# LSH attention and mixture of experts on one core: rows kept in two float16 parts, expert operands turned by the DMA crossbar, five-step weight turns

## The reference

```python
q_bits = (np.einsum('bhsd,dk->bhsk', q, proj) > 0)      # k alike; 6 bits give a bucket
mask = q_bucket[:, :, :, None] == k_bucket[:, :, None, :]
scores = np.where(mask, scale * q @ k.T, -1e9)
attn = softmax(scores);  x = attn @ v                    # rows of all heads: (2, 768, 512)

logits = x @ w_gate                                      # 8 experts
local_gate = sigmoid(x @ w_local)
for s in range(S):                                       # for each batch entry
    e = argmax(logits[s]) if s == 0 or local_gate[s] < 0.5 else prev_e
    h = np.maximum(x[s] @ w1[e], 0.0)                    # 512 -> 1024
    out[s] = softmax(logits[s])[e] * (h @ w2[e])         # 1024 -> 512
```

## Time and profile before

| what | value |
|---|---|
| median of 3 runs | 520.87 us (520.6 to 522.49) |
| the profiled execution | 521.36 us, its span 519.6 us |
| mean granted TensorE clock | 0.971 |
| busy: TensorE, VectorE, ScalarE, GpSimd | 94%, 56%, 57%, 64% of the span |
| chain that ended last | PE 62%, POOL 12%, ACT 10%, DVE 5%, issue 5%, DMA 2% |

### The profile page before, as it was taken

One profiled execution on the slowest core, in us unless ns is written; L12 is line 12 of the kernel. 1 busy time (PEld: TensorE's weight loads), 2 busy tenths in 40 slices (PEclk: granted clock), 3 DMA queues, 4 the chain that ended last, 5 costly groups with the idle time before them and its releaser, 6 DMA issues.

```text
span 519.6 us, 11257 instructions
## 1 busy us (share of the span) xinstructions
PE 486.6 (94%) x4396; PEld 296.3 (57%) x4396; DVE 289.0 (56%) x421; ACT 294.8 (57%) x275; POOL 329.9 (64%) x179
## 2 busy tenths in 40 slices
PE   6889999799999999998878799999999999999994
PEld 2457767477676766676753455555555555555551
DVE  5776566456566666653758554455445554455451
ACT  3278878667868787887874330768585675000000
POOL 1248868849796978879361893499696969500001
PEclk9999999799999999999957999999999999999998
DMA  7665766236563623200092325646638280200000
GB/s 196 149 167 142 215 161 161 74 90 161 161 162 94 183 58 78 50 4 2 9 358 91 100 80 171 257 171 237 232 122 314 60 330 22 112 13 20 7 1 0
DMA packets 54979, 65.11 MB, mean 125 GB/s; under 512 B 30531, under 2 KB 39119, under 8 KB 54930
## 3 DMA queue, kind: packets, MB, share of 16 engines
q1 hardware_dynamic: 45438, 44.22, 28.4%
q10 hardware_dynamic: 6452, 12.05, 7.7%
q0 software_dynamic: 3040, 8.13, 5.0%
HBM read 47.99 MB, written 8.13 MB: 108 GB/s over the span
## 4 chain that ended last, share of the span: by engine, by line
PE 62%; POOL 12%; ACT 10%; DVE 5%; issue 5%; DMA 2%; SPq 1%; ACTq 0%; DVEq 0%; POOLq 0%
PE pA L1254 18%; PE pO L1254 18%; POOL room L505 7%; ACT room L710 5%; POOL W L374 4%; PE pB L1287 3%; ACT room L716 3%; PE pA L578 2%; PE pA L577 2%; PE pB L595 2%; PE pB L594 2%; DMA room<-in_k 1%; PE pP L1244 1%; ACT W L366 1%; PE pO L637 1%
## 5 line engine op out<-in xcount | busy, mean ns | idle before, releaser
L505 POOL TENSOR_TENSOR room<-room 128x1536 f16<-128x1536 f32 x46 | 142.6, 3103 | 56.9 <-ACT room L716 56.7
L374 POOL TENSOR_TENSOR W<-room,W 128x1024 f16<-128x1024 f32 x64 | 135.4, 2135 | 30.9 <-ACT W L366 29.6
L804 DVE TENSOR_REDUCE room<-pA 128x2 f32<-128x1536 f32 x46 | 80.8, 1757 | 51.5 <-PE pA L578 51.3
L360 ACT ACTIVATE room<-W 128x1024 f32<-128x1024 f32 x64 | 64.8, 1048 | 75.1 <-DMA W<-in_moe_w 43.4
L1254 PE MATMUL pA<-W,room 128*128 x432 | 96.2, 379 | 0.4 <-DVE room L1341 0.4
L1254 PE MATMUL pO<-W,room 128*128 x432 | 96.3, 379 | 0.0
L710 ACT ACTIVATE room<-pB 128x1536 f32<-128x1536 f32 x48 | 69.4, 1445 | 43.4 <-PE pB L595 41.4
L716 ACT ACTIVATE room<-room 128x1536 f16<-128x1536 f32 x48 | 71.2, 1484 | 1.5
L1254 PEld LDWEIGHTS pA<-W,room 128*128 128x128 f16 x432 | 42.3, 98 | 47.5 <-issue 0.7
L1254 PEld LDWEIGHTS pO<-W,room 128*128 128x128 f16 x432 | 42.3, 98 | 46.9
L366 ACT ACTIVATE W<-room 128x1024 f16<-128x1024 f32 x64 | 64.9, 1049 | 0.8
(11 more groups left out here) (206 smaller groups left out, 664.7 us busy)
## 6 DMA issues: line engine op xcount, KB each, us to landing
W<-in_moe_w SPq DMA_DIRECT2D x24, 1024.0 KB, 9.6
room<-room SPq DMA_DIRECT2D x93, 96.0 KB, 2.2
W<-in_moe_w ACTq DMA_DIRECT2D x8, 1024.0 KB, 5.8
room<-in_q SPq DMA_DIRECT2D x16, 192.0 KB, 3.4
W<-in_v ACTq DMA_DIRECT2D x4, 768.0 KB, 5.7
x_rows<-XN SPq DMA_DIRECT2D x12, 256.0 KB, 3.4
room<-in_k SPq DMA_DIRECT2D x15, 192.0 KB, 3.9
room<-room SPq DMA_DIRECT2D x31, 18.0 KB
```

The costliest lines, as they stand in the source:

```text
L374: pool.tensor_tensor(parts(r)[:, 1, cols], FULL[:, place(r), cols], parts(r)[:, 0, cols], ALU.subtract).then_inc(s_ready, 1)
L505: pool.tensor_tensor(PTL[:, n % NP, :, :], E32[:, n % 2, :, :], PTH[:, n % NP, :, :], ALU.subtract).then_inc(s_lo, 1)
L804: dve.reduce_max(RM[:, g % 2, 2 * p:2 * p + 2], scores_in(n)[:, :].rearrange("p (i s) -> p i s", i=2), AX.X).then_inc(s_rmax, 1)
```

## The change

1. `norm` writes XN as two float16 parts, already scaled: the result stays in PSUM, then a high copy and a low difference go to XNS. That is five dependent instructions where there were three.
2. `turn_rows` turns both parts (eight float16 transposes into one PSUM block seen as float16), and one copy per row block (`copy_rows`) replaces the high and low instructions; of row blocks 4 to 11 the even ones are copied by ScalarE, the odd ones by VectorE.
3. x_rows holds the float16 parts, so gathered tiles need no split.
4. In the expert stage x and h are turned by DMA transposes that SyncE issues (`turn_x`, one per tile for both parts of x; `turn_h`, one for each part of h; each moves 128 x 1,024 float16, 256 KB). VectorE makes both parts of h before the turn (`split_h`: high part, relu in place in PSUM, low part). TensorE's order becomes up(t+1), down(t). Only the first x and the last h are still turned by TensorE.
5. In attention a weight quarter is split in turns of five steps that begin at step 9; `scale_weights` waits for one half of the low parts at a time; loads go out one head later; the last V split moves from head 3 to head 2. r = 7 is split mostly after the router.
6. The loads of experts 3 to 7 are issued by ScalarE between its splits, two at most in advance, after the down product of the expert's last tile.

```diff
-        V_HEADS, V_SUMS = (-1, 0, 1, 3), (0, 2, 3, 5)
+        V_HEADS, V_SUMS = (-1, 0, 1, 2), (0, 2, 3, 5)
...
+        W_STEPS, W_AT = 5, 9
...
         def turn_rows(pe, i):
...
-            for d in range(DC):
-                last = pe.transpose(pG[buf][:, d * P:(d + 1) * P], XN[:, c, d * P:(d + 1) * P], idf[:, :])
+            for a in range(2):
+                for d in range(DC):
+                    last = pe.transpose(pG[buf][:, a, d * P:(d + 1) * P], XNS[:, c, a, d * P:(d + 1) * P], idh[:, :])
...
+        def copy_rows(eng, i):
             _, buf, before = logits_of(i)
+            eng.wait_ge(s_gt, i + 1)
+            wait(eng, s_gl, before)
+            if by_act(i):
+                eng.activation(XTC[:, buf, :, :], pG[buf], ACT.Copy).then_inc(s_gha, 1)
             else:
+                eng.tensor_copy(XTC[:, buf, :, :], pG[buf]).then_inc(s_gc, 1)
...
-            wait(act, s_ready, 2 * (r if r <= EARLY else r - 1))
+            wait(act, s_ready, 2 * (r if r <= EARLY else r - 1) - 1 + half)
...
-                if h > 2 and h % 2 == 1 and p > 0 and h // 2 <= EARLY:
-                    low_weights(pool, h // 2 - 1, p - 1)
+                r, u = (n - W_AT) // W_STEPS, (n - W_AT) % W_STEPS
+                if 0 <= r < EARLY and u >= 3:
+                    low_weights(pool, r, u - 3)
...
-                if p == 2 and h < V_PARTS:
-                    if h == V_RAW:
+                if p == 2 and 0 <= h - 1 < V_PARTS:
+                    if h - 1 == V_RAW:
                         act.wait_ge(s_vl, NG)
-                    load_weights(act, h)
-                r, u = (h - 2) // 2, (h - 2) % 2 * PAIRS + p
+                    load_weights(act, h - 1)
+                r, u = (n - W_AT) // W_STEPS, (n - W_AT) % W_STEPS
...
-                dst = XN[:, :, :].rearrange("p (j b) n -> p j (b n)", j=J)[:, :, g * D:(g + 1) * D]
-                dve.tensor_tensor(dst, po[:, :, 0:D], REC[:, :].unsqueeze(2).to_broadcast([P, J, D]),
-                                  ALU.mult).then_inc(s_x, 1)
+                chain.link(dve.tensor_tensor(po[:, :, 0:D], po[:, :, 0:D], REC[:, :].unsqueeze(2).to_broadcast([P, J, D]),
+                                             ALU.mult))
+                hi, lo = (XNS.rearrange("p (j b) a n -> p j b a n", j=J)[:, :, g // H, a, g % H * D:(g % H + 1) * D]
+                          for a in range(2))
+                chain.link(dve.tensor_copy(hi, po[:, :, 0:D]))
+                dve.tensor_tensor(lo, po[:, :, 0:D], hi, ALU.subtract).then_inc(s_x, 1)
...
+            def turn_x(t):
+                sp.wait_ge(s_xin[t], 16)
+                wait(sp, s_h, t - 1)
+                sp.dma_start_transpose(XT[:, t % 2, :, :].rearrange("p a (d n) -> p (a d) n", n=P),
+                                       XIN16[:, t, :]).then_inc(s_xt[t % 2], 16)
+
+            def turn_h(t):
+                for a, s in ((0, s_hhi), (1, s_hlo)):
+                    sp.wait_ge(s, t + 1)
+                    wait(sp, s_y, t - 1)
+                    sp.dma_start_transpose(HT[:, t % 2, a, :].rearrange("p (f n) -> p f n", n=P),
+                                           HN[:, a, :]).then_inc(s_ht[a][t % 2], 16)
+
+            turn_x(1)
+            for t in range(NT - 1):
+                turn_h(t)
+                if t + 2 < NT:
+                    turn_x(t + 2)
...
+                pe.wait_ge(s_xt[t % 2], turned(t) - (16 if t % 2 == 0 else 0))
+                wait(pe, s_hlo, t)
...
+                    for a in range(2):
+                        pe.wait_ge(s_ht[a][t % 2], turned(t))
...
-            for t in range(1, NT - 2):
+            for t in range(NT - 2):
                 up(t + 1)
-                xt(t + 2)
                 down(t)
-                ht(t + 1)
...
+                act.wait_ge(s_y, ends[e])
+                r0 = 4 * (e + RING)
+                load_weights(act, r0)
+                for r in range(r0, r0 + 4):
+                    if r + 1 < r0 + 4:
+                        load_weights(act, r + 1)
+                    split_weights(r)
...
+            def split_h(t):
+
                 dve.wait_ge(s_h, t + 1)
...
+                dve.tensor_scalar(HN[:, 0, :], pH[:, 0:F], 0.0, HSC / (XS * WS), ALU.max, ALU.mult).then_inc(s_hhi, 1)
+                dve.tensor_scalar(pH[:, 0:F], pH[:, 0:F], 0.0, HSC / (XS * WS), ALU.max, ALU.mult).then_inc(s_hr, 1)
+                dve.wait_ge(s_hr, t + 1)
...
+                dve.tensor_tensor(HN[:, 1, :], pH[:, 0:F], HN[:, 0, :], ALU.subtract).then_inc(s_hlo, 1)
```

More of the change, by code:

```diff
@@ L276, in logits_of, with by_act, copied @@
             return (i - half) * B + 1, i % 3, i - 1 if i < half + 2 else 0 if i == half + 2 else i - 2
+        def by_act(i):
+            return i >= NS - TAIL and i % 2 == 0
+        def copied(eng, i):
+            if by_act(i):
+                eng.wait_ge(s_gha, sum(by_act(k) for k in range(i + 1)))
+            else:
+                eng.wait_ge(s_gc, sum(not by_act(k) for k in range(i + 1)))
         def turn_rows(pe, i):
             c, buf, before = logits_of(i)
-            wait(pe, s_gc, before)
-            for d in range(DC):
-                last = pe.transpose(pG[buf][:, d * P:(d + 1) * P], XN[:, c, d * P:(d + 1) * P], idf[:, :])
+            if before > 0:
+                copied(pe, before - 1)
+            for a in range(2):
+                for d in range(DC):
+                    last = pe.transpose(pG[buf][:, a, d * P:(d + 1) * P], XNS[:, c, a, d * P:(d + 1) * P], idh[:, :])
             last.then_inc(s_gt, 1)
@@ L1327, in _, with split_weights @@
         def _(act):
-            for r in range(EARLY + 2, NR):
+            def split_weights(r):
                 scale_weights(act, r, 0)
```

206 lines of the change are left out of this document (90 added, 116 removed).

## The result

| | change | before, same session |
|---|---|---|
| median (20 runs each) | 521.91 us | 521.48 us |
| lowest to highest | 510.58 to 540.89 | 519.49 to 526.95 |
| profiled execution, its span | 530.44, 528.4 us | 521.36, 519.6 us |
| mean granted clock | 0.957 | 0.971 |

The forecast was 504.3 us, range 490 to 514. The medians are equal. The ratio is 0.9861 [0.9811, 0.991]; it is taken over each kernel's lowest runs alone, within 1.5% of its lowest, and for the change these are four of the twenty. So the change won some 1.4% when it went well, and nothing in its middle run; instead the runs, 7.5 us apart before, are 30 us apart now. The profiled execution is one of the long ones, 8.5 us above the median. It shows well what goes wrong, but its waits are larger than those of the middle run.

A forecast was written before the change was run, and what follows sets the result against it. TensorE was taken to bound the expert stage and, nearly, attention. The terms -22.1 + 0.9 + 3.4 - 7.5 + 9.3 - 1.1 = -17.1 took 521.36 to 504.3 us, range 490 to 514.

The forecast's parts named there:

- term 1: Expert stage: x and h turns leave TensorE, the cycle falls from 11.67 to 10.37 us; -22.1 us.
- It fits: Expert stage: three DMA turns of 3.4 us each on SP's queue keep up with a 10.37 us cycle.
- rival C: Expert stage: SP's queue does one turn at a time and becomes the bound; 557.5 us at 4.5 us each; chance 0.12.
- rival B: Expert stage: weights come late because turns and loads share DMA engines; +8.6, 512.9 us; chance 0.10.
- Term 2: Entry to the expert cycle: second up product waits for three VectorE instructions, +0.9 us, then a clock fall, +3.4 us.
- The fall of the clock: Entry to the expert cycle: TensorE idles about 3.1 us, then runs at half clock; +3.4 us, bounds 0 and 3.4.
- Term 3: Attention near 90 us: the collision of GpSimd's low parts that idles TensorE goes; -7.5 us, bounds -3 and -7.5.
- nothing of this meets: Attention: with the V split earlier, weight turns from step 9 and half-wise waits, the colliding work no longer coincides; -7.5 us.
- Term 4: Attention heads 1 to 12: longer norm delays hash bits, second hashes stall 0.78 us each; +9.3 us, bounds 5.3 to 10.8.
- Term 5: Rows and router: cheaper row copies shared by ScalarE and VectorE, against a later last norm; -1.1 us, bounds -3 and +1.5.

The follow-up runs named there:

- e1: The change, but loads of experts 3 to 7 move 32 KB instead of 1,024 KB and their scaling reads a constant; 498.01 us.
- e9: e8 without paced loads, with h too turned by TensorE from tile 1 on (16 float16 transposes, one copy); 515.51 us.
- e11: e1 with every DMA turn issued a second time to a spare place, the products waiting for both; 509.71 us.
- e5: The change with x turned by TensorE and an expert's loads sent in two pairs, each after a tile's h turns landed; 517.74 us.
- e6: The change with an expert's loads sent in two pairs, each only when the x turn has landed; 524.25 us.
- e8: e5 plus norm in two parts, gate split moved to head 13, and 14 idle TensorE products before the second up product; 508.78 us.
- e3: The change with norm cut in two: scale, then the hash bits, then the high and low parts; 520.96 us.
- e2: The kernel before with only item 5 of the change (turns of five steps, last V split in head 2); 514.5 us.
- e7: e2 with the gate weights' split moved from head 3 to head 13; 511.04 us.

## Why the prediction was wrong

**The step that failed is in term 1: "It fits".** I priced a turn as one DMA on SP's queue (3.4 us to landing, three in 10.37 us) and the loads as ScalarE's business, and asked of each whether its queue had room. I did not ask what both do on the same 16 engines at once. Measured, turns took 5.1 us in the median and up to 21.1 us to land, and all seven waits in the cycle end with such a landing; without the loads (e1) or nearly without the turns (e9) they are gone. A row to become wary by was there: the earlier trace rows gives the DMA share of the expert stage as 0.55 before, for loads, gathers and scatters. What the trace of before did not have is a turn's own share; it is 0.40 for three a cycle, 1.5 us of all 16 engines for 256 KB (e11 less e1). Turns pay 0.40 for 69 GB/s, loads, gathers and scatters 0.61 for 205: per byte, nearly twice the price. The 0.55 of before becomes 0.55 x 11.67 / 10.36 = 0.62 in the shorter cycle; with 0.40 that is 1.02, a stage with no room to spare; e11 shows that this alone would not have given the size of the waits. The store of 256 KB that I took as the nearest row lands about as fast (3.4 us against 3.2 in e1) and hides this: time to landing of one transfer alone says nothing of how much it occupies. Of rival C I had the effect (TensorE waits for turns) and the wrong resource: SP's queue, with undisturbed issues of 4.9 us in a cycle of 10.36, was not the bound.

The Trainium skill (DMA: Bandwidth & Descriptors, Issuing engines are not separate DMA queues) says that DMAs of all issuing engines end up on the same 16 DMA engines and interleave there. e1 and e9 agree: turns from SP's queue and loads from ScalarE's make no long wait one without the other, and long ones together. I had named the shared engines in rival B, and there only for late weights. The Trainium skill (Advanced Engine Details and Errata, X-Bar Transpose (TRN2)) also calls transposes as fast as regular DMAs; the landing times of one alone agree (3.2 us against 3.4 for the store), the shares above do not.

Measured, term 1 is +11.4 us in the profiled execution, and not -22.1. The middle run is 8.5 us shorter; if all of that lies in this stage, it is +3 there, and e1 (-21.9) is what it would be without the loads beside it.

**Rival B**, weights late at the loads' landing, came in the paced kernels (waits for GpSimd's low part in e5, e6, e8) and once in e3, 3.03 us. In the change's profiled execution TensorE waits for turns alone.

**Term 2** was right in kind: +1.1 us for +0.9. The fall of the clock cost 7.04 - 5.35 = 1.7 us and not 3.4 (2.8 in e6, where that product takes 8.18), and in e1, behind the same idle time of 3.57 us, it did not come at all. The upper bound was taken for the value. What I did not foresee is that waits in the cycle bring the same loss again, five times. Behind the two shortest waits, 1.40 and 0.84 us, it did not come.

**Term 3** was -7.5, measured -7.5 (e2). The step "nothing of this meets" was wrong in itself, since the gate split met GpSimd's low part; the gain without it is -9.9 (e7).

**Term 4** was +9.3, measured +7.9, by the mechanism named: the second hashes wait for bits behind a longer norm. The wait itself is smaller, 0.44 to 0.57 us in eleven heads where I had 0.78 in twelve, in part because the first hashes' wait of 0.4 us goes; 1.7 of the 7.9 are the low clock near 80 us, which I had not forecast here. So that the size came out so close is in part luck: without the clock it is 6.2. The bounds 5.3 to 10.8 held.

**Term 5** was -1.1, measured -2.7, within its bounds: VectorE's float16 copy of 1,024 columns out of PSUM takes 0.69 us, and I had taken 1.22 from the float32 rows. The Trainium skill (VectorE: DVE Perf Modes, Mode 2×_1P) allows two results a cycle for 16-bit data; 0.69 against 1.22 agrees.

**As a whole.** Terms 2 to 5 came to +5.0 in the forecast and to -2.5 in the profiled execution (+1.1 - 0.4 - 2.7 - 0.5, the fall of the clock being counted within the +11.4). Against its forecast the first term is off by 33.5 us, the others together by 7.5 the other way. To the first I gave a chance of 0.22 (B and C) to fail, in forms that it did not take. The range ended at 514 since B, the one case that spoke of shared engines, was priced by a single late load, and late turns beside loads were priced nowhere but in C, as a slower queue.

## What to carry to other kernels

When transfers are added to a stage, add up the DMA share of the stage with theirs, as one does for an engine, and take a sum near 1 as a warning, not as a measure of the waits: e11 ran five cycles at 1.01 without one, e8 waited at 0.90. In this kernel a turn asked nearly twice as much of the 16 engines per byte as loads, gathers and scatters, and its time to landing alone did not show it. Work moved from a full engine to DMA paid where no load was in flight: a split by tile, crossbar turns outside the loads and TensorE turns beside them, together with the repairs in attention, took 3.5% where the whole move took nothing in the middle run. When a kernel's runs lie much further apart than before, look at what its engines share before looking at the mean; here it was the DMA engines.

## What the runs showed of the hardware

- Three DMA turns of 256 KB a cycle add a share of 0.40 for 69 GB/s; loads, gathers and scatters reach 205 GB/s at 0.61. At a share of 1.01 (e11) turns and little else still left TensorE without a wait for 51.8 us.
- A single turn beside loads took up to 21.1 us to land, without them 3.2 in the median and 6.0 at most; SP's pair of issues grows from 3.65 to 12.09 us.
- VectorE's gate split (36 columns, inputs in SBUF) ends with the GpSimd instruction beside it. In the change it starts at 76.84, lasts 2.69 and ends at 79.53, GpSimd's at 76.38 + 3.10 = 79.48; in the kernel before (1.07 us), e7 (2.21) and e8 (1.00) it also ends 0.04 us after GpSimd's. Its second instruction takes 0.20 us where GpSimd is idle and 3.03 beside it (e2). The Trainium skill (GPSIMD Engine Reference, Specifications) tells of contention between the two for VectorE instructions with two SBUF inputs or in a two-port mode; 3.03 (two inputs, e2) and 2.69 (one input, the change) agree in kind.
- Sixteen float16 transposes take TensorE 1.10 us from start to start, eight float32 ones 0.87, for the same numbers turned.
- An idle time of 3.57 us was followed by a product of 5.35 us in e1 and by one of 7.04 in e11: the same pause costs the clock in one execution and not in another.
